# Attention, gated convolution and Fourier mixing on one core: the first batch's convolution moved to TensorE, small VectorE work moved to GpSimd

## The reference

```python
scores = scale * np.matmul(q, k.transpose(0, 1, 3, 2))        # per batch and head, 576 x 576
kth = np.partition(scores, -32, axis=-1)[..., -32:-31]        # the 32 largest of each row stay
attn = softmax(np.where(scores >= kth, scores, -1e9))         # divided by (sum + 1e-9)
x = concat_heads(attn @ v)                                    # (B, S, 512)

gate_pre = sum(conv_w[k] * xp[:, k:k + S, :] for k in range(5))   # causal, per channel
x = (sigmoid(gate_pre) * (x @ w_val)) @ w_out

u = x + real(fft(fft(x, axis=1), axis=2))
un = (u - mean(u)) / sqrt(var(u) + 1e-6)
out = u + relu(un @ w_ch1) @ w_ch2                            # w_ch1 is 512 x 2048
```

## Time and profile before

| | us |
|---|---|
| median of 3 runs | 1170.51 (1168.28 to 1173.09) |
| the profiled execution | 1171.51 |
| its span, first to last instruction | 1169.7 |
| TensorE busy | 1037.2 (89%) |
| VectorE busy | 876.2 (75%) |
| ScalarE busy | 617.2 (53%) |
| GpSimd busy | 403.8 (35%) |

### The profile page before, as it was taken

The page is one execution under the profiler, slowest core; times in us unless marked ns, Lnnn a source line. Parts: engine busy times, 40 slices in busy tenths (PEclk is TensorE's granted clock), DMA queues, the critical chain, the costliest instruction groups (busy, mean ns, idle before and its releaser), DMA issues.

```text
span 1169.7 us, 19830 instructions
## 1 busy us (share of the span) xinstructions
PE 1037.2 (89%) x6608; PEld 827.9 (71%) x6608; DVE 876.2 (75%) x1901; ACT 617.2 (53%) x1253; POOL 403.8 (35%) x703
## 2 busy tenths in 40 slices
PE   3776666589999999999989999999889999999998
PEld 2455555576577888866578888875678888648887
DVE  6999999997998897897998987897988960220000
ACT  3776775555556665644566756555566654012211
POOL 2444452223443422332443423233453222233221
PEclk9987666699999999999999999999999999999999
DMA  7655556011256675620367775411367555207974
GB/s 218 216 179 189 171 175 219 21 31 57 68 186 217 242 259 207 205 67 21 114 220 255 250 231 190 155 57 52 139 221 248 207 205 198 95 1 287 342 273 164
DMA packets 81188, 200.37 MB, mean 171 GB/s; under 512 B 8384, under 2 KB 26560, under 8 KB 81088
## 3 DMA queue, kind: packets, MB, share of 16 engines
q1 hardware_dynamic: 80928, 198.81, 50.3%
q10 hardware_dynamic: 160, 0.30, 0.1%
HBM read 177.58 MB, written 21.50 MB: 170 GB/s over the span
## 4 chain that ended last, share of the span: by engine, by line
PE 39%; issue 27%; POOL 14%; DVE 12%; ACT 4%; DMA 2%; SPq 1%; POOLq 0%; DVEq 0%; ACTq 0%
PE p_m L490 12%; PE p_m L596 10%; PE p_m L582 10%; DVE rest L780 5%; POOL hid_lo L995 3%; DVE top L786 3%; PE p_t L463 2%; POOL bias L931 2%; PE p_t L479 2%; POOL bias L930 2%; PE p_s L450 2%; ACT prob L663 2%; DMA u<-w_ch 1%; POOL x_new L942 1%; POOL q_st L919 1%
## 5 line engine op out<-in xcount | busy, mean ns | idle before, releaser
L786 DVE MAX8 top<-rest 128x8 f32<-128x576 f32 x432 | 304.7, 747 | 0.0
L780 DVE MATCH_REPLACE8 rest<-top,rest 128x576 f32<-128x576 f32 x288 | 211.7, 743 | 0.0
L995 POOL TENSOR_TENSOR hid_lo<-hid,hid_hi 128x256 fp32r<-128x256 f32 (+1 forms) x128 | 104.7, 818 | 303.6 <-ACT hid_hi L725 303.6
L596 PE MATMUL p_m<-w_st,hid_hi 128*128 128x512 f32 x640 | 202.3, 397 | 1.5 <-POOL hid_lo L995 1.5
L582 PE MATMUL p_m<-un_hi,w_st 128*128 128x320 f32 (+1 forms) x1024 | 165.9, 304 | 13.4 <-ACT hid_hi L725 9.6
L663 ACT ACTIVATE prob<-s_sb,bias 128x576 f32<-128x576 f32 x144 | 111.1, 772 | 108.0 <-POOL bias L931 107.8
L463 PE MATMUL p_t<-id_sb,prob 128*128 128x128 f32 x720 | 118.8, 300 | 52.1 <-ACT prob L668 29.9
L582 PEld LDWEIGHTS p_m<-un_hi,w_st 128*128 128x128 f32 x1024 | 143.1, 189 | 26.5 <-issue 23.6
L656 ACT ACTIVATE s_sb<-p_s 128x576 f32<-128x576 f32 x144 | 93.0, 646 | 95.0 <-PE p_s L450 94.8
L479 PE MATMUL p_t<-pT,v_sb 128*64 128x128 f32 (+1 forms) x1600 | 111.5, 292 | 33.9 <-issue 17.8
L450 PE MATMUL p_s<-k_hi,q_st 128*128 128x512 f32 (+1 forms) x320 | 116.2, 366 | 24.2 <-ACT s_sb L656 14.5
(11 more groups left out here) (84 smaller groups left out, 1581.9 us busy)
## 6 DMA issues: line engine op xcount, KB each, us to landing
w_st<-w_split SPq DMA_DIRECT2D x256, 512.0 KB, 4.5
w_split<-w_st SPq DMA_DIRECT2D x32, 512.0 KB, 3.0
k_raw<-kT SPq DMA_DIRECT2D x62, 144.0 KB, 3.0
q_raw<-qT SPq DMA_DIRECT2D x60, 144.0 KB, 2.9
u<-w_ch SPq DMA_DIRECT2D x32, 256.0 KB, 3.4
v_sb<-v SPq DMA_DIRECT2D x16, 256.0 KB, 3.7
wslot<-w_val SPq DMA_DIRECT2D x4, 1024.0 KB, 5.4
wslot<-w_out SPq DMA_DIRECT2D x4, 1024.0 KB, 5.4
```

The source lines that it names most:

```text
L596: mm = pe.matmul(mbank(j), h[i % 2][:, P * j:P * j + P], w2_st[i % NB2][:, w, :], start=f == 0 and part == 0, stop=f == FC - 1 and part == 2)
L780: dve.match_replace(rest[tt % 2][:, :], top[tt % NK][:, 8 * n - 8:8 * n], src[:, :], LOWEST).then_inc(s_chain, 1)
L786: found = dve.max(top[tt % NK][:, 8 * n:8 * n + 8], rest[tt % 2][:, :])
L995: pool.tensor_tensor(hid_lo[i % 2][:, 0:WIDTH[g]], hid[:, 0:WIDTH[g]], hid_hi[i % 2][:, 0:WIDTH[g]].bitcast(F32), ALU.subtract).then_inc(m ...
```

## The change

Four edits, all in the order of work and in who does it.

1. The first batch's convolution goes from VectorE to TensorE. GpSimd makes 20 diagonal matrices of 128x128 out of the identity and the taps' weights (5 a chunk, slots 11 to 14, in buffers not yet in use). TensorE adds up five products a half chunk of 288 tokens, in banks 1 and 2: 8 groups of 5 matmuls in slots 15, 17, 24, 26, 33, 35, 42, 43. ScalarE's tanh reads PSUM and stands in slots 18, 27, 36, 43. The other batches' convolutions stay on VectorE.
2. The reciprocals of all batches go from VectorE to GpSimd, as the first thing of each odd slot, ahead of the biases; the division is a power of -1 over two columns.
3. The low halves of the second head of pairs 1 to 4 (slots 6, 15, 24, 33) go from VectorE to GpSimd, at the end of the slot. Later pairs stay on VectorE.
4. The waits follow: `s_diag` and `s_conv` are new, and the value step with j = 2 of the first batch waits for all four tanh.

```diff
+CONV_BANK = [1, 2]
+DIAG_AT = {11: 0, 12: 1, 13: 2, 14: 3}
+CONV0_AT = {15: (0, 0), 17: (0, 1), 24: (1, 0), 26: (1, 1), 33: (2, 0), 35: (2, 1), 42: (3, 0), 43: (3, 1)}
+TANH0_AT = {18: 0, 27: 1, 36: 2, 43: 3}
...
+        diags = [ab[:, :], un[0][:, :], un[1][:, :], u[2][:, :], u[3][:, :]]
...
+                def convolve(c, o):
+                    pe.wait_ge(s_x, 5 * c + (5 if o else 3))
+                    if o == 0:
+                        pe.wait_ge(s_diag, TAPS * (c + 1))
+                        if c:
+                            pe.wait_ge(m_tanh, c)
+                        else:
+                            pe.wait_ge(s_feat_ev, KC)
+                    for k in range(TAPS):
+                        mm = pe.matmul(mbank(CONV_BANK[o], HALF_S), diag(c, k),
+                                       x_new[c][:, k + o * HALF_S:k + o * HALF_S + HALF_S], start=k == 0, stop=k == TAPS - 1,
+                                       skip_group_check=True)
+                    if o:
+                        mm.then_inc(s_conv, 1)
...
                     if unit_due(s):
                         attend(s - ATTEND)
+                    if s in CONV0_AT and s != CONV_LAST:
+                        convolve(*CONV0_AT[s])
...
+                        act.wait_ge(s_conv, c + 1)
+                        at = BANK * CONV_BANK[0]
+                        act.activation(gate[:, c, :].rearrange("p (o n) -> p o n", o=2),
+                                       p_m[:, at:at + 2 * BANK].rearrange("p (o n) -> p o n", o=2)[:, :, 0:HALF_S],
+                                       ACT.Tanh).then_inc(m_tanh, 1)
...
-                    if due(s, RECIP) and (s - RECIP) % 2:
-                        reciprocal(s - RECIP)
...
-                    if split_at(s, LOW0, LOW) and split_at(s, LOW0, LOW)[1] == 1:
-                        split_low(split_at(s, LOW0, LOW)[0])
+                    p, h = split_at(s, LOW0, LOW) or (0, 0)
+                    if p > POOL_PAIRS and h == 1:
+                        split_low(p)
...
+                def split_low_odd(p):
+                    pool.wait_ge(s_hi, 5 * (p + 1))
+                    whole = (S // P) * P
+                    q, k, high = q_st[1][p % 2], k_lo[1][p % 2], k_hi[1][p % 2]
+                    q_in, k_in = raw(p, 1)
+                    for to, of in ((slice(0, whole), slice(0, whole)), (slice(whole + REST, SP), slice(whole, S))):
+                        pool.tensor_tensor(q[0:D, to], q_in[0:D, of], q[0:D, to].bitcast(F32),
+                                           ALU.subtract).then_inc(s_lo[1], 1)
+                    pool.tensor_tensor(k[:, :], k_in, high[:, :].bitcast(F32),
+                                       ALU.subtract).then_inc(s_lo[1], 1)
...
+                def reciprocal(t):
+
+                    pool.wait_ge(s_exp, t + 1)
+                    if t >= NK:
+                        pool.wait_ge(s_pv, unit_of(t - NK) + 1)
+                    c = slice((t - 1) % NK, (t - 1) % NK + 2)
+                    pool.tensor_scalar(rinv[:, c], psum_row[:, c], EPS_SUM, 2.0, ALU.add, ALU.mult).then_inc(s_radd, 1)
+                    pool.wait_ge(s_radd, t // 2 + 1)
+                    pool.tensor_tensor(rinv[:, c], rinv[:, c], power[:, 1:3], ALU.pow).then_inc(s_rinv, 1)
...
+                def make_diags(c):
+                    pool.wait_ge(s_resid, 80)
+                    pool.wait_ge(s_const, 16)
+                    for k in range(TAPS):
+                        pool.tensor_scalar(diag(c, k), id_sb[:, :], cw_sb[:, c, k:k + 1], None, ALU.mult).then_inc(s_diag, 1)
...
+                    if due(s, RECIP) and (s - RECIP) % 2:
+                        reciprocal(s - RECIP)
                     if due(s, EXPONENT):
                         biases(s - EXPONENT)
...
+                    if s in DIAG_AT:
+                        make_diags(DIAG_AT[s])
...
+                    p, h = split_at(s, LOW0, LOW) or (0, 0)
+                    if p and h == 0:
+                        split_low(p)
+                    elif p and p <= POOL_PAIRS:
+                        split_low_odd(p)
```

More of the change, by code:

```diff
@@ L21 @@
 NS = 6
-FILLS = 19
+FILLS = 20
 TOPK = 32
@@ L42 @@
 XW = TAPS - 1 + S
-HALF = 256
+HALF, HALF_S = 256, S // 2
 ORDER = list(range(1, HALF + 1)) + list(range(S - 1, S - 1 - HALF, -1)) + list(range(HALF + 1, S - HALF)) + [0]
@@ L84 @@
 HIGH_Q, HIGH_K, LOW = {0: 0, 4: 1}, {1: 0, 5: 1}, {2: 0, 6: 1}
+POOL_PAIRS = PAIRS
 HIGH_Q0, HIGH_K0, LOW0 = {2: 0, 5: 1}, {3: 0, 5: 1}, {3: 0, 6: 1}
@@ L88 @@
 NB1, NB2 = 4, 3
+CONV_BANK = [1, 2]
+DIAG_AT = {11: 0, 12: 1, 13: 2, 14: 3}
+CONV0_AT = {15: (0, 0), 17: (0, 1), 24: (1, 0), 26: (1, 1), 33: (2, 0), 35: (2, 1), 42: (3, 0), 43: (3, 1)}
+CONV_LAST = max(CONV0_AT)
+TANH0_AT = {18: 0, 27: 1, 36: 2, 43: 3}
 CONV_AT = {21: [(0, (0, 1))], 22: [(0, (2, 3))], 23: [(0, (4,))], 28: [(1, (0, 1))], 29: [(1, (2, 3))], 30: [(1, (4,))],
@@ L139, in build @@
         id_sb = sb("id_sb", [P, P])
-        power = sb("power", [P, 1])
+        power = sb("power", [P, 3])
         q_raw = sb("q_raw", [P, S])
@@ L195, in build @@
         s_zero = sem("s_zero")
+        s_diag = sem("s_diag")
+        s_conv = sem("s_conv")
         s_feat_mm = sem("s_feat_mm")
@@ L290, in conv_due @@
         def conv_due(s):
-            return [(b, c, taps) for b in range(B) for c, taps in CONV_AT.get(s - NT * b, [])]
+            return [(b, c, taps) for b in range(1, B) for c, taps in CONV_AT.get(s - NT * b, [])]
         def tanh_due(s):
-            return [(b, TANH_AT[s - NT * b]) for b in range(B) if s - NT * b in TANH_AT]
+            return [(b, TANH_AT[s - NT * b]) for b in range(1, B) if s - NT * b in TANH_AT]
         def part_tile(i):
@@ L299, in part_tile, with diag @@
             return w2_st[(i - FC) % NB2][:, :, :]
+        diags = [ab[:, :], un[0][:, :], un[1][:, :], u[2][:, :], u[3][:, :]]
+        def diag(c, k):
+            n = TAPS * c + k
+            return diags[n // 4][:, P * (n % 4):P * (n % 4) + P]
         def u_row(r):
@@ L512, in values @@
                         pe.wait_ge(m_gv, upto_gv(b, j - 3))
+                    elif j == 2 and b == 0:
+                        pe.wait_ge(m_tanh, KC)
                     n0, n1 = VAL[half]
@@ L624, in _ @@
                         feature_weights(FEAT_SLOTS.index(s))
+                    if s == CONV_LAST:
+                        convolve(*CONV0_AT[s])
                     for x in plan[s][0:1]:
@@ L696, in gate_tanh @@
                 def gate_tanh(b, c):
-                    act.wait_ge(m_conv, TAPS * (KC * b + c + 1))
-                    act.activation(gate[:, c, :], gate[:, c, :], ACT.Tanh).then_inc(m_tanh, 1)
+                    if b:
+                        act.wait_ge(m_conv, TAPS * (KC * (b - 1) + c + 1))
+                        act.activation(gate[:, c, :], gate[:, c, :], ACT.Tanh).then_inc(m_tanh, 1)
+                    else:
+                        act.wait_ge(s_conv, c + 1)
[3 more added lines that the diff above has]
+                                       ACT.Tanh).then_inc(m_tanh, 1)
                 def step(what, b, n):
@@ L737, in _ @@
                         store_pT(s - TRANSPOSE)
+                    if s in TANH0_AT:
+                        gate_tanh(0, TANH0_AT[s])
                     if due(s, EXPONENT):
@@ L803, in split_low @@
                                       ALU.subtract).then_inc(s_lo[1], 1)
[L805 to L813, removed]
                 def conv(b, c, taps):
@@ L817, in conv @@
                     dve.wait_ge(s_x, 5 * (p + 1))
-                    if c == 0 and b:
+                    if c == 0:
                         dve.wait_ge(m_z, 3 * b)
-                    elif c == 0:
-                        dve.wait_ge(s_feat_mm, KC)
-                        dve.wait_ge(s_resid, 80)
                     for k in taps:
@@ L893, in _ @@
                     dve.memset(part[:, WIDTH[1]:].bitcast(F32), 0.0).then_inc(s_zero, 1)
-                dve.memset(power[:, :], -0.5).then_inc(s_zero, 1)
+                dve.memset(power[:, 0:1], -0.5).then_inc(s_zero, 1)
+                dve.memset(power[:, 1:3], -1.0).then_inc(s_zero, 1)
                 dve.wait_ge(s_hi, 1)
@@ L972, in deviation @@
                     pool.wait_ge(m_var, NR * b + r + 1)
-                    pool.tensor_tensor(rstd[0:m, r, 1:2], rstd[0:m, r, 0:1], power[0:m, :], ALU.pow).then_inc(m_rstd, 1)
+                    pool.tensor_tensor(rstd[0:m, r, 1:2], rstd[0:m, r, 0:1], power[0:m, 0:1], ALU.pow).then_inc(m_rstd, 1)
                 def step(what, b, n):
```

2 lines of the change are left out of this document (removed).

## The result

The changed kernel took 1206.14 us in the median (1204.80 to 1207.98, 4 runs) against 1171.39 us before: a ratio of 1.0297, 95% interval 1.0281 to 1.0313. The sign was forecast as the likelier one, the time lies 25 us above the forecast and 10 us above the range.

The account below looks back on a forecast made before the run. VectorE was taken to bound the first batch, with a ring through GpSimd close beneath, and TensorE the rest. Terms: +26 us to slot 34, -15.5 us to slot 48, zero after, +10.5 us: 1181 us, range 1152 to 1196.

Parts of the forecast that it names:

- The second bound beneath VectorE: Slots with weight splits: a ring of stations through GpSimd's weight split and bias, 4.35 us a slot, 4.9 with additions.
- Rival 1: VectorE was the bound and GpSimd has room: its additions hide in idle time, 1148 us; chance 0.22.
- diagonals: Slots 11 to 14: 20 GpSimd instructions of 0.42 us ahead of the next biases, +8.4 us (6 to 9.7).
- TensorE's groups: Convolution on TensorE before slot 34: late after full attends in slots 17 and 26, +4 us (0 to 6).
- To slot 34: Slots 5 to 33: reciprocals, low halves, diagonals and convolution on TensorE, less waits that go, sum to +26 us.
- reciprocals, with the waits that go: Slots 7 to 33: reciprocals ahead of biases +10.5 us (8 to 15); two TensorE waits for VectorE's reciprocal go, -5 us.
- low halves: Slots 6, 15, 24, 33: three subtractions on GpSimd, 3.1 us each time, less two bias stalls: +8 us (6 to 10).
- Slots 34 to 48: VectorE bounds here before the change; relieving it gains 14 us plus 1.5 us of TensorE idle time: -15.5 us (-19 to -10).
- The rest: From slot 48: TensorE bounds, GpSimd's 1.0 us in odd slots is mostly covered; zero, -6 to +12 us over three batches.
- Rival 3: Slower throughout: GpSimd's reciprocal ahead of a bias in the middle stage, 4 us a batch, 1193 us; chance 0.13.
- The Trainium skill's rule on the shared interface: GpSimd's SBUF interface contends with VectorE instructions of two SBUF inputs; a several-microsecond gain from moving the convolution was not adopted.

Follow-up runs that it names:

- u_recip: The changed kernel with the reciprocals of all batches back on VectorE: 1181.4 us, 25 us less than the changed kernel.
- u_split: The changed kernel with the second heads' low halves back on VectorE: 1198.3 us, 8 us less than the changed kernel.
- u_conv: The changed kernel with the first batch's convolution and tanh as before, no diagonals: 1187.3 us, 19 us less than the changed kernel.
- d_spread: The changed kernel with the 20 diagonals made one a slot in slots 6 to 25, in GpSimd's idle time: 1193.7 us, 12.5 us less.
- c_one: The changed kernel with TensorE adding one convolution tap of five in the first batch (result lacks the others), diagonals kept: 1194.6 us, 11.6 us less.
- b_split: The kernel before with only the second heads' low halves of pairs 1 to 4 moved to GpSimd: 1172.5 us, ratio 1.0005.
- r_late: The changed kernel with GpSimd's reciprocal behind the biases of its slot instead of ahead of them: 1202.5 us, 4 us less.
- r_mid: The changed kernel with GpSimd's reciprocal half a slot earlier, between the biases and the weight split: 1181.9 us, 24 us less.

## Where the prediction was right and where it failed

**What bounds the kernel: right.** The second bound beneath VectorE is there: the change lengthened slots 5 to 33, the bias wait rose over 40 us (46.0), and VectorE waits, as the forecast wanted to see. Rival 1, VectorE's 36 us as a gain, is refuted by u_recip, u_split and u_conv.

The profiled execution is 33.3 us longer where +10.5 was forecast. The 22.8 us between them fall on three stages: 5.8 to slot 34, 8.0 from there to slot 48, 9.0 behind it. Three steps failed, beside a low price for the diagonals: TensorE's groups were priced at half, the waits for reciprocals were booked as gone, and GpSimd's late reciprocal was put at nothing in the middle stage.

**To slot 34: near the sum, by terms that miss both ways.** Forecast +26 us, measured 31.8. What each run gives back by slot 34, against the forecast's terms:

| term | forecast | run | by slot 34 |
|---|---|---|---|
| reciprocals, with the waits that go | 10.5 - 5 = 5.5 | u_recip | 11.7 |
| low halves | 8 | u_split | 2.1 |
| diagonals | 8.4 | d_spread | 8.9 |
| TensorE's groups | 4 | c_one (four fifths of them) | 8.3 |

The four add up to 31.0 of the 31.8 us. That 26 came so near is in part luck: the low halves cost less than forecast, the groups and the waits more.

**Diagonals: mis-sized.** Forecast 0.42 us, bounds 0.30 to 0.484 us; of the changed kernel, the groups by shape (the L1010 row stands for the three of its kind, with means of 604, 619 and 626 ns):

```profile
L987 POOL TENSOR_TENSOR rinv<-rinv,power 128x2 f32<-128x2 f32 x72 | 55.2, 767 | 6.0
...
L1010 POOL TENSOR_SCALAR un<-id_sb,cw_sb 128x128 f32<-128x128 f32 x8 | 4.8, 619 | 0.0
...
L968 POOL TENSOR_TENSOR k_lo<-k_raw,k_hi 128x576 fp32r<-128x576 f32 x4 | 5.7, 1417 | 0.0
L966 POOL TENSOR_TENSOR q_st<-q_raw,q_st 64x512 fp32r<-64x512 f32 x4 | 5.1, 1277 | 0.0
```

They took 0.60 to 0.63 us, so 12.4 us and not 8.4. Spread over idle time they give 8.9 us by slot 34 and 12.5 us in the medians. The upper bound was wrong in kind: one tensor with a column as operand is slower here than two tensors.

**Reciprocals: price right, path short.** The pair takes 1.0 us, as forecast (0.19 + 0.73 and gaps), the power 767 ns of 571 to 920. That only a quarter of the slots hide them is not in the rows: the earlier trace rows has 17 bias waits in 37 slots. And +10.5 us went by the bias alone. The attend of the same slot waits as well; I had booked -5 us for two of TensorE's waits that go (6.9 us before slot 34), and three of 11.3 us stand there, now for GpSimd.

**Low halves: price right, the total by luck.** 1.28 + 0.32 + 1.42 = 3.0 us each, forecast 3.1. Undoing them gave 8 us over the whole kernel, but the forecast had its +8 us before slot 34, where the runs show 2.1 us (u_split) and 5.2 us (b_split, on the kernel before).

**Convolution on TensorE: mis-sized, by a misreading.** I took the x8 in the earlier trace rows for eight products. It is four: each product of this type is two matmul instructions. A group of five taps is ten. Slot 35 of the changed kernel, on TensorE:

```profile
227.52 2.40 PE L496 MATMUL p_t<-pT,v_sb 128*64 128x128 f32 x20 [0.79 <-ACT pT L715]
...
230.28 2.29 PE L527 MATMUL p_m<-x_new,un 128*128 128x288 f32 x4
...
232.36 1.98 PE L527 MATMUL p_m<-x_new,u 128*128 128x288 f32 x6
```

From 230.28 to 234.34 us are 4.1 us, not 1.3 to 2.4, and the scores of slot 36 stand behind them. At full clock a group takes 2.6 to 2.7 us (slots 42 and 43).

**Slots 34 to 48: outside its bounds, mostly by the groups' price.** Forecast -15.5 us (-19 to -10), measured 31.8 to 24.3, -7.5 us. The forecast gave the chain 47.5 us from slot 34 to slot 44: ten slots of 4.3 us and 4.5 us for three groups. It needs 53.3. The pace was right: from slot 36 to 42, without groups, it is 25.1 us, 4.2 a slot. The three groups are 4.1 + 2.7 + 2.6 = 9.4 us, 4.9 of the 5.8 us that are missing. As an experiment this is weaker: c_one, nearly free of the groups, needs 51.0 us, 2.3 less. It is slower elsewhere: 26.6 us from slot 36 to 42, and in slot 34 its mask waits 3.5 us for a bias behind the low halves. So it stays open how much of the 9.4 us the time would lose without the groups.

**The rest: inside its bounds, but the overlap was wrong.** Forecast 0 (-6 to +12), measured +9.0; a period is 256.5 us from slot 79 to slot 115 where the kernel before has 252.2, outside the 2 us allowed. The forecast called GpSimd's 1.0 us covered by asking when the bias and the transpose are needed, and never asked the same of the attend, which needs the reciprocal in its own slot. Rival 3 has the size, 4 us a batch for a measured 3, and it wasn't an alternative to the forecast but came on top of it. Its mechanism, the reciprocal ahead of the bias, is not what the runs show: r_late takes it away and loses as much. r_mid, where the attend doesn't wait for it and the next bias hardly does, loses nothing.

The Trainium skill's rule on the shared interface (GPSIMD Engine Reference, Specifications), which the prediction weighed, has some support: in the first batch, with VectorE's two-input convolution and low halves gone, GpSimd's second bias instruction goes from a mean of 396 ns (40 to 236 us) to 299 ns (changed kernel, 40 to 265 us), and the keys' low halves, 1521 ns in the earlier trace rows, take 1417 ns. But a mean also moves where VectorE's two-input work is the same: from 527 to 779 us that bias instruction takes 340 ns in the kernel before and 382 ns in r_mid. So it depends on which instructions meet as well, and the runs give the rule no price.

## What to carry to other kernels

An engine that is busy half the time can still hold the pace, if others wait at a fixed place in its order: look at what the consumer's wait ends with and what the engine did just before, not at its share. Do this for every consumer of what is moved; here the bias was looked at and the attend was not. Before moving work there, find the engine's own idle gap and put the work into it; the same instructions cost 24 us at the head of the slot and nearly nothing in the gap. And where two bounds lie within some per cent, price parts together, since one relief pays for only so many additions.

## What the runs showed of the hardware

GpSimd's power takes 575 ns over one column and 767 ns over two. Its product of a 128x128 tensor with a column takes 604 to 626 ns, its product of two 128x128 tensors 494 ns.

A late GpSimd also costs by way of TensorE's clock. In slot 8 of the changed kernel TensorE stands idle for 5.1 us, and the chain of eight matmul instructions behind it, on the same shapes, takes 6.0 us at a granted clock of 0.59, where the kernel before took 3.6 us at 1.00. The granted clock was 1.00 up to 44.4 us, where TensorE fell idle, and 0.50, its level of 1.2 GHz, from 46 to 53.7 us. The length of the idle time does not settle it alone: in u_split it is 2.2 us there, and the chain takes 5.98 us; in the kernel before it is 1.1 us. TensorE in the changed kernel, then in the kernel before:

```profile
49.55 1.33 PE L480 MATMUL p_t<-id_sb,prob 128*128 128x128 f32 x5 [5.12 <-ACT prob L707]
...
50.68 6.04 PE L507 MATMUL p_m<-gv,gate 128*128 128x512 f32 x8
```

```profile
46.76 3.60 PE L490 MATMUL p_m<-gv,gate 128*128 128x512 f32 x8
```
